# Gated linear attention and two feed-forward layers on one core: products of y in output tiles of 64 channels where they fit

## The reference

```python
# q, k, v, f_logit: (4 batches, 8 heads, 768 steps, 48 channels), float32
f = 1.0 / (1.0 + np.exp(-f_logit))
state = np.zeros((B, H, D, D), dtype=np.float32)
for t in range(S):
    state = f[:, :, t, :, None] * state + np.einsum('bhd,bhe->bhde', k[:, :, t], v[:, :, t])
    y[:, :, t] = np.einsum('bhd,bhde->bhe', q[:, :, t], state)
x = y as (3072 tokens, 384)
h = x @ moe_w_in                                    # 384 to 2048
x = np.where(h > 0, h, np.exp(np.minimum(h, 0)) - 1) @ moe_w_out
out = np.maximum(x @ moe2_w_in, 0) ** 2 @ moe2_w_out
```

## Time and profile before

| what | value |
|---|---|
| median of three runs | 997.84 us (995.43 to 998.28) |
| the profiled execution, its own time | 997.89 us |
| span of its instructions | 995.9 us |
| TensorE busy with matmuls | 961.6 us, 97% of the span |
| TensorE weight loads | 820.2 us |
| VectorE, ScalarE, GpSimd busy | 495.5, 391.1, 277.4 us |
| mean granted clock of TensorE | 0.995 of full speed |

### The profile page before, as it was taken

One profiled execution on the slowest core, in us unless ns is written; L12 is line 12 of the kernel. 1 busy time (PEld: TensorE's weight loads), 2 busy tenths in 40 slices (PEclk: granted clock), 3 DMA queues, 4 the chain that ended last, 5 costly groups with the idle time before them and its releaser, 6 DMA issues.

```text
span 995.9 us, 27529 instructions
## 1 busy us (share of the span) xinstructions
PE 961.6 (97%) x11972; PEld 820.2 (82%) x11972; DVE 495.5 (50%) x700; ACT 391.1 (39%) x685; POOL 277.4 (28%) x221
## 2 busy tenths in 40 slices
PE   5789989999999999999999999999999999999998
PEld 4668767887888778788878879999999999999997
DVE  5878675575657666573325663333333333333332
ACT  2735633443534343453444453232332332322322
POOL 2236454454536454444423541000000000000000
PEclk9989999999999999999999999999999999999999
DMA  6743313303030212111003321000010000000000
GB/s 204 211 124 93 107 40 109 86 14 96 35 98 22 77 55 77 60 50 50 2 2 109 97 76 68 1 33 32 1 63 0 32 32 0 32 32 0 32 1 32
DMA packets 54187, 56.88 MB, mean 57 GB/s; under 512 B 19520, under 2 KB 46400, under 8 KB 54080
## 3 DMA queue, kind: packets, MB, share of 16 engines
q1 hardware_dynamic: 51232, 43.86, 15.4%
q10 hardware_dynamic: 2848, 11.44, 3.1%
HBM read 45.84 MB, written 9.44 MB: 56 GB/s over the span
## 4 chain that ended last, share of the span: by engine, by line
PE 90%; DVE 3%; issue 3%; ACT 2%; DMA 2%; ACTq 0%; DVEq 0%
PE ps L1536 8%; PE ps L1535 8%; PE ps L1540 8%; PE ps L1574 7%; PE ps L1573 7%; PE ps L1577 7%; PE ps L1183 6%; PE ps L1071 6%; PE ps L1206 5%; PE ps L1185 5%; PE ps L1192 5%; PE ps L1208 5%; PE ps L1212 5%; PE ps L1133 2%; PE ps L1106 1%
## 5 line engine op out<-in xcount | busy, mean ns | idle before, releaser
L1489 DVE TENSOR_TENSOR g<-g 128x512 f32<-128x512 f32 x96 | 67.1, 699 | 264.0 <-ACT g L1409 264.0
L1409 ACT ACTIVATE g<-ps 128x512 f32<-128x512 f32 x112 | 67.1, 599 | 284.6 <-PE ps L1540 280.3
L669 POOL TENSOR_TENSOR glo<-g,ghi 128x512 fp32r<-128x512 f32 x80 | 111.2, 1390 | 234.7 <-ACT ghi L502 234.7
L876 DVE SCALAR_TENSOR_TENSOR g<-e,g 128x512 f32<-128x512 f32 x80 | 63.0, 788 | 142.6 <-ACT g L496 142.6
L1535 PE MATMUL ps<-xhi,wts 128*128 128x512 f32 x336 | 131.9, 393 | 0.7 <-ACT xhi L487 0.7
L1536 PE MATMUL ps<-xhi,wts 128*128 128x512 f32 x336 | 131.9, 393 | 0.0
L1574 PE MATMUL ps<-wts,ghi 128*128 128x384 f32 x380 | 128.9, 339 | 0.0
L1573 PE MATMUL ps<-wts,ghi 128*128 128x384 f32 x380 | 127.6, 336 | 0.0
L495 ACT ACTIVATE e<-ps 128x512 f32<-128x512 f32 x80 | 47.8, 598 | 166.1 <-PE ps L1192 166.1
L1183 PE MATMUL ps<-xhi,wts 128*128 128x512 f32 x240 | 99.6, 415 | 0.7 <-ACT g L496 0.7
L1540 PE MATMUL ps<-xlo,wts 128*128 128x512 f32 x336 | 95.3, 392 | 0.0
(11 more groups left out here) (123 smaller groups left out, 1576.4 us busy)
## 6 DMA issues: line engine op xcount, KB each, us to landing
raw<-w SPq DMA_DIRECT2D x52, 192.0 KB, 2.6
q<-qk SPq DMA_DIRECT2D x22, 256.0 KB, 4.4
gate<-fl SPq DMA_DIRECT2D x10, 512.0 KB, 5.0
k<-qk SPq DMA_DIRECT2D x10, 512.0 KB, 3.7
x<-xo ACTq DMA_DIRECT2D x6, 768.0 KB, 3.3
xs<-x ACTq DMA_DIRECT2D x6, 768.0 KB, 4.3
out<-PT SPq DMA_DIRECT2D x24, 192.0 KB, 1.9
v<-vn SPq DMA_DIRECT2D x11, 384.0 KB, 3.6
```

The lines of the kernel that those rows point to most:

```text
L669: nc.gpsimd.tensor_tensor(out=glo[:, f % 2, :], in0=g[:, f % 2, :], in1=ghi[:, f % 2, :].bitcast(F32), op=ALU.subtract).then_inc(s_glo, 1)
```

## The change

The twelve blocks of 32 output channels are taken in pairs where a head's 48 channels begin on an even block, so that the pair is one aligned stretch of 64 partitions: head 0 of pairs 0 and 2, head 1 of pairs 1 and 3. Such a head is done in one matmul with 64 stationary columns in place of two with 32. The other heads stay with two of 32. All with 64 come first in each part of `q_state` and each z of `values`, and then those with 32. In `last_column` the order for each batch is four with 64, then four with 32.

`q_state` has 12 matmuls in each part in place of 16 (4 with 64 columns, 8 with 32), `values` 24 for each z in place of 32 (8 and 16), `last_column` 16 in place of 24 (8 and 8): 88 in place of 120 in a unit.

```diff
-    def shares(group):
-        for m in range(KD):
-            a, third = divmod(4 * m + group, 3)
-            for j in range(2):
-                if third == 1 or third == 2 * j:
-                    yield m, a, j, third
+    def shares(j):
+        def tiles(a):
+            first, n = 3 * a + j, 32 if (3 * a + j) % 2 else 64
+            return [(a, *divmod(32 * i, P), n, 32 * i - 96 * a) for i in range(first, first + 2, n // 32)]
+        return [tiles(j) + tiles(j + 2), tiles(1 - j) + tiles(3 - j)]
...
             for i in range(2):
-                for group in range(4):
-                    for j in range(2):
-                        m, a, _, third = [x for x in shares(group) if x[2] == j][i]
+                for both in zip(shares(0)[i], shares(1)[i]):
+                    for j, (a, m, at, n, channel) in enumerate(both):
                         u, rows = j ^ part, slice(HP * j, HP * j + D)
                         last = nc.tensor.matmul(
-                            pair(c, h, "Y")[32 * group:32 * group + 32, u, m * CELL:m * CELL + C],
-                            state[rows, 2 * (h % 2) + u, 2 * a * D + 32 * third:2 * a * D + 32 * third + 32],
+                            pair(c, h, "Y")[at:at + n, u, m * CELL:m * CELL + C],
+                            state[rows, 2 * (h % 2) + u, 2 * a * D + channel:2 * a * D + channel + n],
                             queries(c, h)[rows, u * PAIRS + a, 0:C],
...
-            for i in range(4):
-                for group in range(4):
-                    m, a, j, third = list(shares(group))[i]
+            for i, j in ((0, 0), (0, 1), (1, 0), (1, 1)):
+                for a, m, at, n, channel in shares(j)[i]:
...
-                            vz[rows, h % 2, z, a, 32 * (third + j):32 * (third + j) + 32], blocks,
+                            vz[rows, h % 2, z, a, channel + 32 * j:channel + 32 * j + n], blocks,
...
-                for block in range(4 * KD):
-                    m, group = divmod(block, 4)
+                for block, n in ((0, 64), (6, 64), (4, 64), (10, 64), (2, 32), (3, 32), (8, 32), (9, 32)):
+                    m, at = divmod(32 * block, P)
                     a = block // 3
...
-                                            state[:, 2 * (h % 2) + u, 32 * block:32 * block + 32],
+                                            state[:, 2 * (h % 2) + u, 32 * block:32 * block + n],
```

More of the change, by code:

```diff
@@ L1099, in q_state @@
                 pe.wait_ge(s_u, count(c, h, 1, 1))
-            begun_groups = set()
             for i in range(2):
-                for group in range(4):
-                    for j in range(2):
-                        m, a, _, third = [x for x in shares(group) if x[2] == j][i]
+                for both in zip(shares(0)[i], shares(1)[i]):
+                    for j, (a, m, at, n, channel) in enumerate(both):
                         u, rows = j ^ part, slice(HP * j, HP * j + D)
                         last = nc.tensor.matmul(
-                            pair(c, h, "Y")[32 * group:32 * group + 32, u, m * CELL:m * CELL + C],
-                            state[rows, 2 * (h % 2) + u, 2 * a * D + 32 * third:2 * a * D + 32 * third + 32],
+                            pair(c, h, "Y")[at:at + n, u, m * CELL:m * CELL + C],
+                            state[rows, 2 * (h % 2) + u, 2 * a * D + channel:2 * a * D + channel + n],
                             queries(c, h)[rows, u * PAIRS + a, 0:C],
-                            start=(part == 0 and (u, group) not in begun_groups), stop=False, skip_group_check=True)
-                        begun_groups.add((u, group))
+                            start=(part == 0 and i == 0), stop=False, skip_group_check=True)
             if part:
@@ L1133, in values @@
                         last = nc.tensor.matmul(
-                            banks[32 * group:32 * group + 32, u, m * CELL + HP * z:m * CELL + C],
-                            vz[rows, h % 2, z, a, 32 * (third + j):32 * (third + j) + 32], blocks,
-                            start=(fresh and z == 0 and i == 0), stop=(z == 1 and i == 3), skip_group_check=True)
+                            banks[at:at + n, u, m * CELL + HP * z:m * CELL + C],
+                            vz[rows, h % 2, z, a, channel + 32 * j:channel + 32 * j + n], blocks,
+                            start=(fresh and z == 0 and (i, j) == (0, 0)), stop=(z == 1 and (i, j) == (1, 1)),
+                            skip_group_check=True)
             if z:
@@ L1162, in last_column @@
             for u in range(UB):
-                for block in range(4 * KD):
-                    m, group = divmod(block, 4)
+                for block, n in ((0, 64), (6, 64), (4, 64), (10, 64), (2, 32), (3, 32), (8, 32), (9, 32)):
+                    m, at = divmod(32 * block, P)
                     a = block // 3
-                    last = nc.tensor.matmul(pair(c, h, "Y")[32 * group:32 * group + 32, u, m * CELL + C:(m + 1) * CELL],
-                                            state[:, 2 * (h % 2) + u, 32 * block:32 * block + 32],
+                    last = nc.tensor.matmul(pair(c, h, "Y")[at:at + n, u, m * CELL + C:(m + 1) * CELL],
+                                            state[:, 2 * (h % 2) + u, 32 * block:32 * block + n],
                                             q_last[:, h % 2, u * PAIRS + a:u * PAIRS + a + 1],
```

## The result

The changed kernel takes 1005.18 us (median of four, 1004.50 to 1006.14), the kernel before beside it 996.63 us. The ratio is 1.0086, 95% interval 1.0064 to 1.0108: slower by 8.6 us. A second comparison gave 1.0104 (1.0077 to 1.0131), medians 1005.30 and 995.59 us. The forecast was 1007.5 us, slower, from a sum of +9.9 us. The direction was right, and so were the mechanisms in the steady units. Two terms of the sum were off with opposite signs: the units by +1.2 us, chunk 0 by about -3 us.

The account below looks back on a forecast made before the run. TensorE was taken to bound the kernel: 7.9 (eight units) + 1.0 (chunk 1) + 1.4 - 0.4 (chunk 0) = +9.9 us on 997.89 gives 1007.8; predicted 1007.5 us, own range 1004 to 1011.5, eight in ten 1001 to 1013.

Parts of the forecast that it names:

- What bounds the kernel: From chunk 2 on TensorE is busy nearly throughout, so added time there moves the end by as much.
- Wide records with 128 moving columns gain nothing: `q_state` and `values` z = 0: a 64-column record takes about 27 ns, twice a narrow one; gain zero.
- `last_column` costs 0.52 us a unit: `last_column`: wide records at 29 ns add 0.19 us, three changes of shape 0.33 us a unit.
- A change of shape costs 0.11 us: TensorE, eight added changes a full unit: each costs 0.11 us, ends 0.08 and 0.13; together 0.88 us.
- The unit: +0.99 us forecast: Full unit: 8 x 0.11 - 0.08 + 0.19 = +0.99 us; eight units from chunk 2 on, +7.9 us.
- Chunk 0: +1.4 - 0.4 forecast: Chunk 0: longer `values` and `last_column` +1.4 us; 7% fewer records shorten 5.2 us of instruction waits, -0.4 us.
- the +1.0 of the forecast: Chunk 1's two units, where TensorE also waits for others: half the added cost, +1.0 us, ends 0.4 and 2.0.
- Count decides: Rival, all four stages: the number of records decides and changes are free; about -7.2 us, 990.7 us; chance 0.10.
- `last_column` by count: Rival: changes cost, but `last_column` goes by record count, -0.14 for +0.19 us a unit; +6.3, 1004.1 us; chance 0.14.
- Cheap changes from 64 to 32: Rival: 64-to-32 changes cost much less, only 2 of 8 remain, `last_column` by count; 998 us, within 0.3%; chance 0.08.
- The clock: Rival: gaps thin out the y stages, each of eight units gets a half-clock stretch; +13.6 more, 1021 us; chance 0.06.

Follow-up runs that it names:

- the all-wide kernel: Changed kernel with every head at 64 columns in `q_state` and `values`, and the old `last_column`; ratio to the kernel before 0.9903.
- The all-wide last column: Kernel before with `last_column` alone changed to six matmuls of 64 columns for each batch; ratio to the kernel before 0.9999.
- level 5 with 33 columns: Kernel before with 33 stationary columns in place of 32 in the products of level 5; ratio to the kernel before 0.9993.
- Three fewer: Changed kernel with the same matmuls reordered in `last_column` and `values` z = 0, three changes of shape fewer in a unit; ratio to the kernel before 1.0047.

## Why the prediction was right, and which terms were off

**What bounds the kernel: right.** From chunk 2 on the period moved by what TensorE's stages moved (1.13 in the stages, 1.14 in the period). No other engine took a part of it.

**Wide records with 128 moving columns gain nothing: right.** 26 ns against 12.9, and the all-wide kernel has 0.67 us for `q_state` with half the records.

**`last_column` costs 0.52 us a unit: right.** 0.49 to 0.50 measured in the stage, 0.45 in the period. The all-wide last column shows the price of the columns alone, 29 ns a record. That it is the weight load which sets this price is read from how it goes with the stationary columns; no run changes the load by itself. One reading of the prediction was wrong here: the rows of 32, 48 and 62 columns don't share a moving width, as `new_state` with 48 columns has 48 moving. Those of 32 and 62 columns do (32 moving), and the all-wide run and level 5 with 33 columns carry the point without the third. The rule of the Trainium skill on a fixed overhead ("TensorEngine Tiling (Array Packing)", Instruction Overhead) does not describe this stream: the trace disagrees, with half the records taking 0.29 us longer.

**A change of shape costs 0.11 us: right in size, from three sides.** Three fewer give 0.31 us; one fewer gives 0.08 in the kernel before; the bare pause is 0.10. The rule of the Trainium skill that changing the tiling mode drains the engine ("TensorEngine Tiling (Array Packing)", Key Properties) fits all three.

**The unit: +0.99 us forecast, 1.14 measured.** The surplus is in `q_state`, 0.15 and 0.14 us a part in place of 0.11 (the second is 0.27 less the 0.13 of the change ahead of `values`), in that change, and around z = 1, 0.08 in place of 0.03. The row of z = 1 itself is 0.01 us shorter, not 0.03 longer; what grew is the idle time between it and `last_column`, from 0.06 to 0.15 us, also where `last_column` is narrow again. Why is open. For `q_state` one more thing shows: where the first wave is wide, the slowest records take longer than the 293 ns of the earlier trace rows:

```profile
L1105 PE MATMUL ps<-q,state x24: 269/282/321, 236.1 to 236.6; 48*32 48x128 f32 x16, 48*64 48x128 f32 x8
```

321 ns, 28 more. I read this as the longer load of 64 columns, which is not made ahead after a change either; no run shows it by itself. I had priced the changes that the diff adds, but not that the changes which were there before now enter a wider tile. In all the term was 0.15 us too small, about a sixth; eight units make it +9.1 in place of +7.9 us.

**Chunk 0: +1.4 - 0.4 forecast, -2.1 and -1.8 us measured.** This step failed. I had taken 7% off the 5.2 us of waits, in proportion to the records of a whole unit; in the stages at the end of chunk 0 the records fall by 27%, from 352 to 256, and even that would have given only -1.4 us. In fact most of the waits went: 0.8 us is left in the first profile after, 1.5 in the second. The kernels with wide records in chunk 0 reach `hidden` at 51.4 to 55.6 us, the profiles with narrow ones at 56.3 to 56.7, also where the wide ones stand in `last_column` alone. The direction is the same in all of them; the size is not settled. It holds a part of clock (1.00 ahead of `hidden` in three of these kernels, 0.50 in the others), and the run with the change in chunk 0 alone differs by 1.1 us from the changed kernel with the same matmuls up to there. That TensorE waits there for its own instructions is my reading: the profile says only that nothing which it shows was waited for. Wide records both last longer and are fewer instructions, and no run separates the two.

**Chunk 1 and the later waits.** The first profile of before has waits of 0.61 us near 350 and 0.93 near 420; the profile after has neither. By the periods around them (46.27 and 46.66 in place of 45.4) they cost 2.1 us. Chunk 1 can be read by itself, from the first `hidden` to the `new_state` of unit (2,0), less the 0.15 us of the one `q_state` part of unit (2,0) in it: 189.05 - 56.63 = 132.42 us before and 190.31 - 54.50 = 135.81 after, so +3.2 us in the first profiles. The second profiles have 186.90 - 56.34 = 130.56 and 186.33 - 54.55 = 131.78, so +1.1 us. The two first profiles differ by 6.8 us of half clock between 140 and 154 us, where the second ones have none. So I take +1.1 for the change, near the +1.0 of the forecast, and put the other 2 us down to the clock, as 3.4 us of half clock cost 1.6 us above. The whole accounts, in us:

| pair of profiles | chunk 0 | chunk 1 | eight units | later waits and rest | span |
|---|---|---|---|---|---|
| first (995.9, 1004.0) | -2.1 | +3.2 | +9.1 | -2.1 | +8.1 |
| second (992.9, 1000.2) | -1.8 | +1.1 | +9.1 | -1.1 | +7.3 |
| forecast | +1.0 | +1.0 | +7.9 | 0 | +9.9 |

**The rivals.** Count decides: refuted, stage by stage, though it may have a true core at the start of the program, where fewer and wider records left less waiting. `last_column` by count: refuted. Cheap changes from 64 to 32: refuted by 0.20 us at that very place. The clock: refuted where it was placed, as the granted clock is 1.00 in all eight units from chunk 2 on, before and after. In chunk 1 its stretches moved between profiles of one program (one near 141 us in one of the two of before; one near 140 and one at 147 us in one of the two of after) and were not brought by the change.

So the forecast came out near the time partly by luck: +1.2 us in the units stood against about -3 us in chunk 0, and waits of 1 to 2 us in the later units, which the prediction didn't have, went away as well.

## What to carry to other kernels

Count what a matmul occupies, not matmuls. With small tiles either the moving columns or the weight loads keep the array full; a tile of twice the columns has half as many tiles beside it and, when it is full, about 1.7 times the price by columns here (58 ns for 35). Before mixing tile shapes, count the changes of shape along TensorE's order, about 0.1 us each here, and group equal shapes, or pad a shape by one column to match its neighbour. And read a change of a few microseconds from the period of a steady unit and from two profiles of each kernel: a total of 0.9999 hid +0.29 us a unit.

## What the runs showed that was not expected

- The end of chunk 0 changes by up to 5 us (first `hidden` at 56.6 or 51.4 us) where only the shape and number of TensorE's matmuls differ; some 0.8 us of it is clock, and the same matmuls gave 54.5 us in one kernel and 55.6 in another.
- Two profiles of one program differ by 3 us in span (995.9 and 992.9; 1004.0 and 1000.2), mostly through stretches of 3.4 or 6.8 us at half clock in chunk 1 that are there in one and not in the other. In the steady units they agree to 0.02 us.
